# Linear attention, a dense gated layer and a routed expert layer on one core: expert weight pieces issued by the sync engine in place of GpSimd

## The reference

```python
# 1. attention with a delta rule, B=4, H=8, S=768, D=48
k_n = k / (norm(k) + 1e-6)
for t in range(S):
    y[t] = q[t] @ state
    state += beta[t] * outer(k_n[t], v[t] - k_n[t] @ state)
# 2. dense gated layer on x = y, 3072 tokens, 384 -> 1536 -> 384
x = ((x @ w_a) * (x @ w_b)) @ w_out
# 3. one of 8 experts per token, 384 -> 1024 -> 384
logits = x @ w_gate + modality_bias[modality_id]
e = argmax(logits); g = softmax(logits)[e]
out = g * (relu(x @ w1[e]) @ w2[e])
```

## Time and profile before

| | before |
|---|---|
| runs | 1091.69, 1093.02, 1096.7 us |
| profiled execution, its own time | 1091.77 us |
| its span, first to last instruction | 1089.8 us |
| PE busy | 974.7 us, 89% of the span |
| DVE busy | 508.5 us, 47% |
| POOL busy | 323.7 us, 30% |
| ACT busy | 298.1 us, 27% |
| mean granted TensorE clock | 0.94 |
| q0 (issued by POOL) | 114.65 MB in 32800 packets, 32.1% of sixteen DMA engines |
| q1 (issued by SP) | 53.94 MB in 118256 packets, 19.7% |

### The profile page before, as it was taken

How to read it: one execution, slowest core, us unless ns; L and a number is a source line. 1 busy time by engine, 2 the same in 40 slices (tenths; PEclk the granted TensorE clock), 3 DMA queues, 4 the chain that set the end, 5 groups by cost and what they waited for, 6 DMA issues and landing times.

```text
span 1089.8 us, 27301 instructions
## 1 busy us (share of the span) xinstructions
PE 974.7 (89%) x10964; PEld 841.9 (77%) x10965; DVE 508.5 (47%) x1098; ACT 298.1 (27%) x552; POOL 323.7 (30%) x589
## 2 busy tenths in 40 slices
PE   2264999999999998999999999999946999999995
PEld 2253787888788887888888788888845999999995
DVE  3865665466545654556445553333374222222221
ACT  2022232233322332323323223222310222222221
POOL 1112134333243332433333334332311122222221
PEclk8656999999999999999999999999975999999998
DMA  8594357755675576655765565443537611172110
GB/s 237 163 217 156 93 175 214 222 162 179 180 204 172 180 211 177 207 173 167 212 167 169 157 180 164 151 153 114 167 105 257 217 44 43 37 240 69 43 43 23
DMA packets 151160, 170.10 MB, mean 156 GB/s; under 512 B 109567, under 2 KB 115841, under 8 KB 151056
## 3 DMA queue, kind: packets, MB, share of 16 engines
q0 software_dynamic: 32800, 114.65, 32.1%
q1 hardware_dynamic: 118256, 53.94, 19.7%
HBM read 99.34 MB, written 69.40 MB: 155 GB/s over the span
## 4 chain that ended last, share of the span: by engine, by line
PE 80%; DVE 8%; DMA 6%; issue 2%; ACT 1%; POOL 1%; SPq 0%; DVEq 0%; POOLq 0%; ACTq 0%
PE bank L487 20%; PE bank L489 18%; PE bank L488 18%; PE bank L533 3%; PE bank L415 2%; PE bank L447 2%; PE bank L663 2%; PE bank L403 2%; PE bank L457 2%; PE bank L433 2%; DVE work L960 2%; PE bank L477 2%; PE bank L467 2%; DMA work<-we_in 2%; DVE work L964 1%
## 5 line engine op out<-in xcount | busy, mean ns | idle before, releaser
L487 PE MATMUL bank<-wbuf,x_hi 128*128 128x512 f32 (+1 forms) x582 | 247.9, 426 | 3.5 <-DVE x_lo L1287 1.3
L489 PE MATMUL bank<-wbuf,x_lo 128*128 128x512 f32 (+1 forms) x582 | 230.6, 396 | 0.0
L488 PE MATMUL bank<-wbuf,x_hi 128*128 128x512 f32 (+1 forms) x582 | 230.4, 396 | 0.0
L718 ACT ACTIVATE work<-bank 128x512 f32<-128x512 f32 (+1 forms) x193 | 105.1, 545 | 348.3 <-PE bank L489 198.9
L1356 POOL DMA_DIRECT2D expert_split_scratch<-work x128 | 70.3, 549 | 428.3 <-DVE work L1008 416.2
L487 PE MATMUL bank<-wbuf,g_hi 128*128 128x384 f32 (+1 forms) x488 | 173.1, 355 | 5.3 <-DVE g_lo L1297 2.6
L489 PE MATMUL bank<-wbuf,g_lo 128*128 128x384 f32 (+1 forms) x488 | 164.9, 338 | 0.0
L488 PE MATMUL bank<-wbuf,g_hi 128*128 128x384 f32 (+1 forms) x488 | 164.6, 337 | 0.0
L1008 DVE TENSOR_TENSOR work<-work 128x384 fp32r<-128x384 f32 x128 | 70.9, 554 | 144.6 <-ACT work L718 144.6
L487 PEld LDWEIGHTS bank<-wbuf,x_hi 128*128 128x128 f32 x582 | 111.0, 191 | 28.3 <-issue 2.9
L489 PEld LDWEIGHTS bank<-wbuf,x_lo 128*128 128x128 f32 x582 | 110.7, 190 | 26.0
(11 more groups left out here) (143 smaller groups left out, 1242.7 us busy)
## 6 DMA issues: line engine op xcount, KB each, us to landing
expert_split_scratch<-work POOLq DMA_DIRECT2D x256, 192.0 KB, 2.7
work<-we_in POOLq DMA_DIRECT2D x128, 192.0 KB, 3.4
work<-a_in POOLq DMA_DIRECT2D x24, 896.0 KB, 6.9
wbuf<-expert_split_scratch SPq DMA_DIRECT2D x24, 768.0 KB, 6.2
work<-wm_in POOLq DMA_DIRECT2D x18, 384.0 KB, 4.9
inverse_in_scratch<-work SPq DMA_DIRECT2D x24, 256.0 KB, 2.9
work<-a_in SPq DMA_DIRECT2D x6, 768.0 KB, 6.2
x_scratch<-work SPq DMA_DIRECT2D x48, 96.0 KB, 2.5
```

Of the source, the lines that this page charges most:

```text
L487: pe.matmul(o, a_hi, w_hi, start=first, stop=False)
L488: pe.matmul(o, a_hi, w_lo, start=False, stop=False)
L489: return pe.matmul(o, a_lo, w_hi, start=False, stop=last)
L718: return act.activation(o, i, ACT.Copy)
```

## The change

The loads and stores of the pieces move from POOL's stream into SP's. The three functions are the same but for the engine. In SP's slot, pieces 0 and 1 come after `store_y2`, and pieces 2 to 5 after `load_t12` and `load_ke`; the first two loads come at the end of slot 1.

```diff
@@ sync engine @@
+            def load_expert_piece(j):
+                sp.wait_ge(S["lo"], ND + max(j - 1, 0))
+                sp.dma_start(raw[:, j % 2, :], we_in[j]).then_inc(s_raw[j % 2], 16)
+
+            def store_expert_piece(j):
+                e, c = j // NS, j % NS
+                sp.wait_ge(S["lo"], ND + j + 1)
+                sp.dma_start(ws_hi[e, c], s_hi[j % 2].bitcast(F32)).then_inc(s_hs[j % 2], 16)
+                sp.dma_start(ws_lo[e, c], s_lo[j % 2].bitcast(F32)).then_inc(s_ls[j % 2], 16)
+
+            def expert_piece(n, i):
+                pieces = expert_pieces(n - 1)
+                if i < len(pieces):
+                    j = pieces[i]
+                    store_expert_piece(j)
+                    if j + 2 < MORE:
+                        load_expert_piece(j + 2)
...
                 if n >= 2:
                     store_y2(n - 2)
+                expert_piece(n, 0)
+                expert_piece(n, 1)
                 if n + 2 < STEPS:
                     load_t12(n + 2)
                 if n % GROUP == 0 and n // GROUP + 3 < GROUPS:
                     load_ke(n // GROUP + 3)
+                for i in range(2, 6):
+                    expert_piece(n, i)
+                if n == 1:
+                    load_expert_piece(0)
+                    load_expert_piece(1)
@@ GpSimd @@
             def slot(n):
                 if n >= 1 and n + 1 < STEPS:
                     v_scale(n + 1)
-                expert_piece(n, 0)
                 if n >= 4 and n % GROUP == 0 and n + 4 < STEPS:
                     triangle(n // GROUP + 1)
-                expert_piece(n, 1)
-                expert_piece(n, 2)
...
                 if n + 2 < STEPS:
                     load_row(n + 2)
-                expert_piece(n, 3)
...
-                if n == 1:
-                    load_expert_piece(0)
-                    load_expert_piece(1)
-                expert_piece(n, 4)
-                expert_piece(n, 5)
```

More of the change, by code:

```diff
@@ L303, in store_y2 @@
                     sp.dma_start(x2[row:row + CH, :], b_y[b * CH:(b + 1) * CH, 0, :]).then_inc(S["ost"], 16)
+            ws_hi = wsplit[:, :, 0:WE].rearrange("e p (n w) -> e n p w", w=SPLIT2)
+            ws_lo = wsplit[:, :, WE:2 * WE].rearrange("e p (n w) -> e n p w", w=SPLIT2)
+            def load_expert_piece(j):
[13 more added lines that the diff above has]
+                        load_expert_piece(j + 2)
             def slot(n):
@@ L1344, in load_dense @@
                 pool.dma_start(raw3[:, i % 3, :], wm_in[:, dense_columns(i)]).then_inc(s_rd[i % 3], 16)
[L1346 to L1365, removed]
             def slot(n):
```

## The result

The changed kernel is slower: 1104.98 us, median of seven runs (1100.27 to 1108.26), against 1093.58 us (1091.69 to 1096.7, seven runs) before. The ratio is 1.0101, with a 95% interval of 1.0078 to 1.0124. The profiled execution took 1108.26 us with a span of 1106.5 us. It is the highest of the seven runs, so its trace shows 16.5 us as lost where the medians show 11.4. Its mean granted clock, 0.930, is also the lowest of the seven (the others have 0.931 to 0.942), so the share of the clock in this trace is rather high.

The account below looks back on a forecast made before the run. PE was taken as the bound, busy 667.78 of 680 us, with at most 3.3 us to gain. Trips -1.5, late slots +3.7 and clock +1.7 made +3.9 on 1091.77, stated as 1096; range 1089.5 to 1107.

Parts of the forecast that it names:

- no change: Whole kernel: a measured time within 0.5%, 5.5 us, of before, from 1087.5 to 1098.5; chance 0.60.
- rival B: Slots 3 to 19: SP is held up as long as now by the four inverse loads' own rows; 13.8 us, 1106; chance 0.20.
- POOL's 384 issues: POOL's stream: 384 fewer issues at 543 ns each free some 209 us, worth nothing since nothing waits for POOL.
- Shorter trips: Low half to landed load: -0.3 us per trip, about five trips in PE's waits, -1.5 us; bounds -3.3 and +5.
- Rival D: Every piece load from SP lands as late as its 256 KB loads, 4.4 us: 1102 to 1106; chance 0.10.
- Late in slots 3, 7, 11, 15 and 19: Piece loads stand behind SP's inverse loads and stores, so PE's line 533 starts late: 3.7 us, bounds 3.7 and 11.4, or 16.
- The relief of 1.7 us: SP's small-row block in these five slots: without POOL's transfers in its middle, SP is free up to 1.7 us sooner.
- 6.33: Time in us from SP's end of line 303 to PE's line 533: 1.08 hand-overs, 3.4 landing, 1.85 from ACT to PE.
- What stands behind the pieces: SP's transfers behind the pieces, load_t12 and the store of line 265, have over a slot, 28 us, of slack: cost nothing.
- a new wait in other slots: Sign of a wrong forecast: PE gets a new wait in slots other than 3, 7, 11, 15 and 19.
- Clock: After PE's 2.2 us wait in slot 19, one stretch at the lower clock: +1.7 us.
- four new ones: 7: Upper bound of the clock cost: four new low-clock stretches after PE waits, 7 us; with none, 0.

Follow-up runs that it names:

- e4: Kernel before, pieces on POOL, but in slots 3, 7, 11, 15 and 19 POOL waits ahead of piece 0 until SP handed over line 303: 1106.44 us, ratio 1.0129.
- e10: Changed kernel with the inverse loads of line 295 issued one per slot in place of four in every fourth: 1095.24 us, ratio 1.0026.
- e1: Changed kernel with the 768 KB load of the keys (load_ke) moved up between pieces 0 and 1: 1097.55 us, ratio 1.0058.
- e11: Changed kernel with the 896 KB load of the attention inputs issued by SP right behind piece 2's stores and load: 1097.21 us, ratio 1.0048.
- e5: Kernel before, pieces on POOL, but in slots 4 and 8 SP waits for piece 1's low half before load_ke: 1092.84 us, ratio 1.001.
- e8: Changed kernel with inverse loads one per slot and load_ke between pieces 0 and 1: 1092.01 us, ratio 1.0004.
- e12: Changed kernel with inverse loads one per slot, load_ke between pieces 0 and 1, and the 896 KB load on SP behind piece 2: 1088.54 us, ratio 0.996.
- e2: Changed kernel with the four inverse loads of line 295 issued behind pieces 0 and 1 in place of ahead: 1110.97 us, ratio 1.0163.

## Why the prediction was right, and where it was wrong

The direction of the sum and the place of its largest term were right, and the time fell into the range. But 1096 was 9 us too low, the time is outside the forecast's own 1091 to 1101, and "no change", which had 0.60, was not what came. The range held only because it took in half of rival B, whose reason the traces refute: that part of the hit was luck. Three terms failed.

- **POOL's 384 issues, nothing:** right. Its earlier start of the 896 KB load, "early enough now", was counted as harmless; see below at what stands behind the pieces.
- **Shorter trips, -1.5 us:** right in sign and near in size. Landing 2.9 us against the 3.4 of the earlier trace rows, PE's wait for `g_lo` at slot ends (line 528) 1.0 against 2.0, and the part from slot 23 to the routing 51.1 us against 52.2. By the Trainium skill, page "DMA: Bandwidth & Descriptors", section "Specifications", the first byte comes some 0.4 us sooner from the sync engine; the trace's 0.5 is near that, though no row separates first byte from landing. Rival D is refuted by the same 2.9.
- **Late in slots 3, 7, 11, 15 and 19, +3.7:** that a late issue makes these slots long is shown by e4 and e10. Its size was wrong: PE's new waits in the five slots are 0.2, 1.4, 0.4, 2.7 and 2.1 us, 6.8 in all against 3.7. Two steps were mis-sized. The relief of 1.7 us was read in slot 11 and taken off in all five. Counted from the start of the slot, SP is done with line 303 0.7, 0.9, 3.1, 0.7 and 2.3 us sooner than before: more than slot 11 could use, and too little in slots 3, 7 and 15. And from the end of line 303 to line 561 it took 6.7, 6.8, 7.0, 7.5 and 7.0 us, not 6.33. About half of the 3.3 us more is landing: 3.1 to 4.4 us in the five slots (4.1 to 5.6 before the change) against the 3.4 that the sum took. Rival B's reason did not come: the stretch that it held to be unchanged took 4.9, 5.5, 4.2, 3.8 and 4.1 us, and 5.6, 6.4, 7.3, 5.0 and 6.0 before. Its 1106 is near the result for other reasons. That the queue is full, as the prediction says, no row shows; the rows show a longer hand-over.
- **What stands behind the pieces, "I cost them at nothing":** this failed. I looked at whether the transfers of the attention part would be in time, and they were. I didn't ask whom they would meet now that they leave later. `load_ke` stood behind pieces 0 and 1 in the diff, and I left it out. The keys and POOL's 896 KB squeeze the load behind piece 2 in slots 4 and 8: 8.5 us to land in slot 4, waits of 1.9 and 1.6 us. The prediction named a new wait in other slots as a sign of being wrong, and it came. Either cure brings both slots back: e1 (keys early) and e11 (896 KB behind the piece). e5 shows that keys that leave 3.4 us late harm nothing by themselves.
- **Clock, +1.7:** the term that was most mis-sized. Seven stretches of 3.4 us more came (two slots had two in a row), 23.9 us at half speed, some 12 us. The bound "four new ones: 7" was too small as well. I priced one wait over 2 us; waits of 1.4 to 1.9 us had such a stretch, too, as two of the three waits of 1.76 us for `w_form` had in the kernel before.

Put together from the trace, the profiled spans differ by 16.7 us: 10.4 us more of PE busy, which the slow clock explains, and 6.3 us more of PE idle. New waits are 9.2 us (line 561: 12.6 against 2.4, less the 1.0 saved at line 528); the other 2.9 us are the balance of many small differences, the largest of them waits for transfers before 120 and after 830 us that became 0.9 and 1.1 us shorter; I did not follow them up.

That the waits cause the slow stretches is likely, but seen only as a coincidence of place, over all fourteen traces: each of the 47 stretches between 165 and 795 us begins within 3 us of the end of a PE wait of 1.3 us or more. Not every wait has one. Of 19 waits over 2 us there, 16 had one begin within 1.8 us of their end, and of 59 between 1.3 and 2 us, 30. What a stretch costs is seen by itself in slot 19 of e11, which kept its wait and had none. It is 3.2 us shorter than in the changed kernel with a wait only 0.4 us shorter, and the stretch of the changed kernel is 6.8 us long there, 3.4 us at half speed. It stays open how the early keys and the inverse load together make slot 8 long in e8 and e12.

The page "DMA: Bandwidth & Descriptors" of the Trainium skill says in its section "Issuing engines are not separate DMA queues" that issuing from several engines at once saves only the time on the sequencer. As a guide to what moving transfers is worth it is too little for this kernel: the kernel with the same transfers took 1.0101 of the time in one order and split of the issues and 0.996 in another. What counts is which transfer stands ahead of which.

## What to carry to other kernels

When transfers move to another engine's stream, write down for each slot what is now ahead of them in the queue, and for each transfer that now stands behind them whom it will meet when it leaves later. A small transfer that is needed at once should stand ahead of a large one that is not, and in the same queue: here that brought slots 4 and 8 back. Take a hold-up slot by slot, not from one slot for all. Give a wait of PE of 1.3 us or more in the middle of dense work a second price for the clock around it, 1.7 us for each stretch of 3.4 us, and a chance: half of the waits up to 2 us had one here, and most of the longer ones.

## What the runs showed of the hardware

- SP hands over a 192 KB transfer in 0.33 to 0.45 us where nothing holds it up, and POOL takes 0.54; behind four loads with 1024 short rows each, the same hand-over by SP took up to 3.23 us in e2.
- With a 768 KB and an 896 KB load under way a 192 KB load landed after 8.5 us (slot 4 of the changed kernel); the fastest one in that kernel landed in 2.3. From 415 to 423 us in slot 11 of the changed kernel the DMA engines were 88.9% busy with SP's queue alone, for 1.53 MB.
- At each of the five PE waits of 1.4 to 2.7 us (slots 4, 7, 8, 15, 19 of the changed kernel) a stretch of 3.4 or 6.8 us at a granted clock of 0.50 began, between 0.9 us before the wait's end and 1.1 us after it. Those in slots 3 and 11, in both kernels, began between 0.1 us before and 1.7 us after the end of a wait of 1.76 us for `w_form`; the same wait in slot 7 of the kernel before had none.
